# Attention output divided by broadcast sums on GpSimd instead of the probabilities, q turned in tile pairs, one unsplit unit, weights split in place

## The reference

```python
q_rot, k_rot = (rotate(q), rotate(k))
scores = scale * np.matmul(q_rot, k_rot.transpose(0, 1, 3, 2))
scores = scores - np.max(scores, axis=-1, keepdims=True)
attn = np.exp(scores)
attn = attn / (np.sum(attn, axis=-1, keepdims=True) + 1e-09)
return np.matmul(attn, v).astype(np.float32)
```

## Time and profile before

| | us |
|---|---|
| median of 3 runs | 1056.86 (1056.76 to 1062.91) |
| the profiled execution's own time | 1058.53 |
| its span, first to last instruction | 1056.7 |

### The profile page before, as it was taken

How to read it: one execution, slowest core, us unless ns; L and a number is a source line. 1 busy time by engine, 2 the same in 40 slices (tenths; PEclk the granted TensorE clock), 3 DMA queues, 4 the chain that set the end, 5 groups by cost and what they waited for, 6 DMA issues and landing times.

```text
span 1056.7 us, 21205 instructions
## 1 busy us (share of the span) xinstructions
PE 998.6 (94%) x7040; PEld 930.8 (88%) x7040; DVE 668.1 (63%) x1330; ACT 567.1 (54%) x1344; POOL 314.9 (30%) x317
## 2 busy tenths in 40 slices
PE   5888999998999998999999999999999999999997
PEld 4777777777888878999999999788999999999997
DVE  6999999999999997978666775455221221221220
ACT  4888999988999996444444442642131131121120
POOL 5777877877676721100000000342000000000000
PEclk9999999999999999999999999999999999999999
DMA  3122222222112101100000000130000000000000
GB/s 90 48 58 59 55 55 60 61 59 56 35 40 47 35 14 48 61 1 0 0 0 0 0 0 0 60 119 2 1 24 23 1 23 22 0 22 20 3 22 22
DMA packets 70078, 32.90 MB, mean 31 GB/s; under 512 B 62496, under 2 KB 63392, under 8 KB 70048
## 3 DMA queue, kind: packets, MB, share of 16 engines
q1 hardware_dynamic: 69760, 32.20, 11.4%
q10 hardware_dynamic: 288, 0.33, 0.1%
HBM read 27.79 MB, written 4.72 MB: 31 GB/s over the span
## 4 chain that ended last, share of the span: by engine, by line
PE 62%; DVE 18%; issue 11%; ACT 7%; DVEq 1%; DMA 0%; ACTq 0%; SPq 0%
PE psum L559 19%; PE psum L561 18%; PE psum L560 18%; DVE row_stats L974 4%; DVE pT_lo L991 3%; ACT probs L756 3%; DVE row_stats L997 2%; DVE probs L1004 2%; DVE pT_hi L991 2%; PE psum L530 1%; DVE qT L955 1%; ACT pT_hi L769 1%; PE psum L544 1%; DVE xT L1013 1%; PE psum L649 1%
## 5 line engine op out<-in xcount | busy, mean ns | idle before, releaser
L932 ACT ACTIVATE h_hi<-psum 128x288 fp32r<-128x288 f32 x96 | 39.5, 411 | 245.8 <-PE psum L561 245.8
L530 PE MATMUL psum<-ident,probs 128*128 128x128 f32 x800 | 138.4, 285 | 30.4 <-ACT pT_hi L769 12.9
L530 PEld LDWEIGHTS psum<-ident,probs 128*128 128x128 f32 x800 | 92.4, 142 | 55.7 <-ACT pT_hi L769 17.3
L974 DVE TENSOR_REDUCE row_stats<-psum 128x1 f32<-128x576 f32 (+1 forms) x160 | 119.9, 749 | 8.0 <-ACT probs L756 4.0
L1178 DVE SCALAR_TENSOR_TENSOR h_lo<-psum,h_hi 128x288 fp32r<-128x288 f32 x96 | 44.0, 458 | 125.8 <-ACT h_hi L932 125.8
L756 ACT ACTIVATE probs<-psum,row_stats 128x576 f32<-128x576 f32 (+1 forms) x160 | 118.8, 743 | 6.2 <-DVE row_stats L974 4.4
L559 PE MATMUL psum<-u_hi,wc_hi 128*128 128x288 f32 x384 | 114.3, 298 | 0.2 <-DVEq L1172 0.2
L559 PE MATMUL psum<-h_hi,wc_hi 128*128 128x288 f32 x384 | 113.7, 296 | 0.0
L560 PE MATMUL psum<-u_lo,wc_hi 128*128 128x288 f32 x384 | 113.3, 295 | 0.0
L560 PE MATMUL psum<-h_lo,wc_hi 128*128 128x288 f32 x384 | 113.3, 295 | 0.0
L561 PE MATMUL psum<-h_hi,wc_lo 128*128 128x288 f32 x384 | 112.9, 294 | 0.0
(11 more groups left out here) (137 smaller groups left out, 2940.1 us busy)
## 6 DMA issues: line engine op xcount, KB each, us to landing
stage_w<-in_moe_w_ch_dram SPq DMA_DIRECT2D x8, 768.0 KB, 4.4
out_dram<-stage_out SPq DMA_DIRECT2D x8, 576.0 KB, 3.7
raw_q<-in_q_dram SPq DMA_DIRECT2D x32, 128.0 KB, 2.2
raw_k<-in_k_dram SPq DMA_DIRECT2D x32, 128.0 KB, 2.3
raw_v<-in_v_dram SPq DMA_DIRECT2D x32, 128.0 KB, 2.1
stage_w<-in_moe_w_k_dram SPq DMA_DIRECT2D x4, 512.0 KB, 3.8
stage_w<-in_moe_w_v_dram SPq DMA_DIRECT2D x4, 512.0 KB, 3.5
raw_v<-in_v_dram SPq DMA_DIRECT2D x64, 16.0 KB, 2.0
```

The costliest lines, as they stand in the source:

```text
L530: ins = t.transpose(bank[:, at:at + P], probs[i][:, tile, at_key:at_key + P], ident[:, :])
L974: d_.tensor_reduce(neg_max[0:m, at:at + 1], score_banks[at][0:m, :, 0:HALF], AX.XY, ALU.max, negate=True).then_inc(maxed, 1)
```

## The change

- The probabilities are no longer divided. The inverse row sums (one `invert` per head, `I0`, all five tiles) go to a DRAM tensor `sum_rows` (`sums_out`, 640 single floats), come back broadcast over 64 partitions (`sums_back`, tile `rb`), and GpSimd multiplies the attention output of a pair of heads in place (`scale_x`, 576 wide, once per pair of slots). `N` steps are gone from both orders; `turn` waits for the exponentials alone.
- q is turned in pairs of tiles (three transposes, with k's tail tile as a fourth, `prepare` unit 0), then k's four full tiles (unit 1): two rounds where there were three (`PREP` 3). ScalarE and VectorE have four P steps each in place of three.
- Only unit 0 is whole; units 1, 4 and 5 are now split.
- q and k lie side by side in `raw_qk`, so GpSimd multiplies both by cos in one 640-wide instruction, and by sin in another.
- Gated weights load straight to where `w1_lo` lies (`w1_raw`) and are split in 20 pieces of 512, the last five after the loop of slots.
- The orders change: `v0` moves behind `E2` on ScalarE; `T1` moves ahead of `S0` on TensorE.

```diff
-    WHOLE = (1, 4, 5)
+    WHOLE = (0,)
-    ORDER = steps("T0 S0 T1 P0 S1 T2 V0 S2 T3 V1 V2 T4 P1 T5 S3 T6 V3 T7 V4 P2 V5 S4 V6 V7")
-    ACT_ORDER = steps("H0 H1 E0 N4 H2 P0 v0 H3 E1 O0 H4 P1 H5 E2 H6 H7 N1 P2 E3 O1 E4")
-    DVE_ORDER = steps("M0 L0 I1 N2 N3 M1 L2 P0 L3 M2 O0 I0 P1 N0 M3 L6 L7 P2 M4 O1")
+    ORDER = steps("T0 T1 S0 P0 S1 T2 V0 T3 V1 S2 T4 V2 T5 S3 P1 T6 V3 T7 S4 V5 V4 V6 V7")
+    ACT_ORDER = steps("H0 H1 P0 P1 P2 H2 E0 H3 E1 H4 O0 H5 E2 v0 H6 H7 P3 E3 O1 E4")
+    DVE_ORDER = steps("I0 M0 L0 L1 M1 P0 L2 P1 L3 M2 P2 L4 O0 L5 M3 L6 L7 M4 P3 O1")
-    LAST_DVE_ORDER = steps("I1 L0 N2 N3 X0 L2 X1 L3 O0 X2 X3 X4 L6 X5 L7 X6 O1 X7")
+    LAST_DVE_ORDER = steps("I0 L0 L1 X0 L2 X1 L3 O0 X2 L4 X3 L5 X4 L6 X5 L7 X6 O1 X7")
 ...
+            def sums_out(it, kk):
+                sp.wait_ge(sum_inv, upto(it, kk, 1, 1))
+                sp.dma_start(sum_rows[bass.ds(it * 2 + kk, 1), :].rearrange("o (t p) -> p (o t)", p=P),
+                             rsums[:, kk % 2, :], allow_slow_non_contiguous=True).then_inc(sums_stored, 16)
+            def sums_back(it, kk, first=False):
+                i = kk % 2
+                sp.wait_ge(sums_stored, it * 32 + (16 * kk + 16))
+                if i == 0 and not first:
+                    sp.wait_ge(x_scaled, it)
+                sp.dma_start(rb[i * D:i * D + D, :], sum_rows[bass.ds(it * 2 + kk, 1), 0:S].to_broadcast([D, S])).then_inc(rb_in, 16)
+            def slots(it, w=None, first=0, tiles=1, more=True, start=False):
+                if not start:
+                    sums_out(it, -1)
+                    next_v(it, 0)
+                    sums_back(it, -1)
+                if w is not None:
+                    load_w1(w, it, first, tiles)
+                if more:
+                    next_qk(it, 0)
+                sums_out(it, 0)
+                next_v(it, 1)
+                sums_back(it, 0, first=start)
+                if more:
+                    next_qk(it, 1)
 ...
+                g.tensor_tensor(times_cos[:, :, :, :], raw_qk[i][:, :, :, :], both(cos), ALU.mult).then_inc(rope_step, 1)
+                g.tensor_tensor(times_sin[:, :, :, :], raw_qk[i][:, :, :, :], both(sin), ALU.mult).then_inc(rope_step, 1)
+                pool.wait_ge(rope_step, upto(it, kk - 1, 2, 2))
+                for j, (rot, done) in enumerate(((rot_q[i], q_roped), (rot_k[i], k_roped))):
+                    g.tensor_tensor(*rope_half(rot, times_cos, times_sin, j, 0), ALU.subtract)
+                    g.tensor_tensor(*rope_half(rot, times_cos, times_sin, j, 1), ALU.add).then_inc(done, 1)
 ...
+            def scale_x(p):
+                pool.wait_ge(span_out, p * 4 + 4)
+                pool.wait_ge(rb_in, p * 32 + 32)
+                at = bass.ds(p * COLS + 1, S)
+                g.tensor_tensor(xT[:, at], xT[:, at], rb[:, :], ALU.mult).then_inc(x_scaled, 1)
 ...
+            def slots(it, n, scaling):
+                split_v(it, 0, 0)
+                rotate(it, 0, 2, False)
+                split_w1_hi(it, n)
+                pool.wait_ge(w_hi, it + 1)
+                split_v(it, 1, 1)
+                split_w1_lo(it)
+                rotate(it, 1, 3, False)
+                if scaling:
+                    scale_x(it - 1)
 ...
+                if unit == 0:
+                    if first:
+                        pe.wait_ge(first_roped, 2)
+                    else:
+                        pe.wait_ge(q_roped, upto(it, kk, 1, 1))
+                        pe.wait_ge(k_roped, upto(it, kk, 1, 1))
+                        pe.wait_ge(prep_lo, upto(it, kk, 4, 0))
+                    for p in range(PAIRS):
+                        t.transpose(prep_bank[:, p * P:(p + 1) * P], rot_q[i][:, 2 * p:2 * p + 2, :].rearrange("p a d -> p (a d)"), ident[:, :])
+                    ins = t.transpose(prep_bank[:, PAIRS * P:PAIRS * P + P], rot_k[i][:, FULL, :, :].rearrange("p a d -> p (a d)"), ident[:, :])
```

More of the change, by code:

```diff
@@ L347, in load_v, with load_w1 @@
                     sp.dma_start(raw_v[i][at:at + TAIL, FULL, 0:D], v_d[bass.ds(head, 1), FULL * P:S, :].rearrange("o p d -> p (o d)")).then_inc(v_in[i], 16)
[L349 to L352 removed]
+            def load_w1(w, it, first, tiles):
                 src = w[bass.ds(it * (tiles * P) + (-first * tiles * P), tiles * P), :].rearrange("(t p) n -> p t n", p=P)
[L354 removed]
@@ L356, in load_pair @@
[L356 to L365 removed]
+                sp.dma_start(w1_raw[:, bass.ds(it * UNIT, UNIT)].rearrange("p (t n) -> p t n", t=tiles), src).then_inc(w1_in, 16)
@@ L373, in _ @@
             sp.wait_ge(first_roped, 2)
-            load_pair(0, w_k, 0, 1, again=False)
+            load_qk(2, 0)
+            sp.wait_ge(k_roped, 2)
+            load_qk(3, 1)
+            slots(0, w_k, 0, 1, start=True)
             with sp.Fori(1, KD) as it:
-                load_pair(it, w_k, 0, 1)
+                slots(it, w_k, 0, 1)
             with sp.Fori(KD, N_WKR) as it:
-                load_pair(it, w_r, KD, 2)
+                slots(it, w_r, KD, 2)
             with sp.Fori(N_WKR, N_WV) as it:
-                load_pair(it, w_v, N_WKR, 2)
-            with sp.Fori(N_WV, HEADS // 2 - 1) as it:
-                load_pair(it)
-            sp.wait_ge(v_used, HEADS - 2)
-            load_v(HEADS - 1, 1)
+                slots(it, w_v, N_WKR, 2)
+            with sp.Fori(N_WV, HEADS // 2 - 2) as it:
+                slots(it)
+            slots(HEADS // 2 - 2, more=False)
+            last = HEADS // 2 - 1
+            sums_out(last, -1)
+            next_v(last, 0)
+            sums_back(last, -1)
+            sums_out(last, 0)
+            sums_back(last, 0)
+            sums_out(last, 1)
+            sums_back(last, 1)
             sp.wait_ge(span_out, 2 * HEADS)
@@ L453, in _ @@
             rotate(0, 1, 1, True)
-            with pool.Fori(0, N_WV) as it:
-                for i, split_w1 in enumerate((split_w1_hi, split_w1_lo)):
-                    split_v(it, i, i)
-                    rotate(it, i, i + 2, False)
-                    split_w1(it)
-            with pool.Fori(N_WV, HEADS // 2 - 1) as it:
-                for i in range(2):
-                    split_v(it, i, i)
-                    rotate(it, i, i + 2, False)
-            for i in range(2):
-                split_v(HEADS // 2 - 1, i, i)
+            def slots(it, n, scaling):
[8 more added lines that the diff above has]
+                    scale_x(it - 1)
+            slots(0, 1, False)
+            with pool.Fori(1, N_WV) as it:
+                slots(it, it + 1, True)
+            with pool.Fori(N_WV, HEADS // 2 - 1) as it:
+                slots(it, N_WV, True)
+            last = HEADS // 2 - 1
+            split_v(last, 0, 0)
+            for n in range(last, HALF_UNITS):
+                split_w1_hi(n, N_WV)
+                pool.wait_ge(w_hi, n + 1)
+                split_w1_lo(n)
+                if n == last:
+                    split_v(last, 1, 1)
+                if n == last + 2:
+                    scale_x(last - 1)
+            scale_x(last)
             for n, (size, sources, hi, lo, _) in enumerate(TOK_UNITS):
```

285 lines of the change are left out of this document (138 added, 147 removed).

## The result

The changed kernel takes 1165.28 us (median of 4 runs, 1164.4 to 1166.16) against 1056.81 for the kernel before, measured beside it: a ratio of 1.101, 95% interval 1.0974 to 1.1047. That is 108 us slower. The profiled execution took 1165.27, its span 1163.1.

A forecast was written before the change was run, and what follows sets the result against it. VectorE was taken to pace the kernel before (slot 12.0 us), a loop through GpSimd the changed one. 15 pairs of 29.25 us plus the ends gave +74.6 on 1058.5, 1133.1; less 1.7, 1131 us, range 1092 to 1166.

The forecast's parts named there:

- rival 4: Half clock in every attention slot, with stalls behind it: B = 8.0, slot pair 30.65, total 1152 us; chance 20%.
- The loop: In attention, P0 waits for values_hi, split_v and the whole rope: slot at least A plus B, pair 29.25 us; 48%.
- A: Part of a slot from the end of v on ScalarE to k roped on GpSimd: 6.70 us, odd heads 7.95.
- B: Part of a slot from TensorE's P0 to the end of the next v on ScalarE: 7.3 us.
- the warm B: B without clock loss: 6.1 us if ScalarE never waits, taken as 6.4 with small stalls.
- about 7 in 10 slots pay: Share of attention slots assumed to lose some 1.3 us in B to TensorE's half clock, giving B = 7.3.
- Ends: Outside the thirty intervals: v(0) +2.7 us, v(30) to v(31) 9.3, then 3.1 to the last half-slot, there -1.5.
- Cost nothing: Loads behind sums_out on SP's queue stay covered: no cost, or 0 to 2 us a pair if that cover went.
- Rival 1: No loop in attention, VectorE relieved: slot 10.7 us, 40 us less, total 1017 us; chance 5%.

The follow-up runs named there:

- the filler: The changed kernel with 24 extra transposes of the identity on TensorE ahead of P0's wait for the rope: 1145.49 us, ratio 1.0845 to the kernel before.

## Why the prediction was right, and where it was off

It said 1131, range 1092 to 1166, slower at 92%; the time is 1165. The mechanism is the one named, and the experiments bear out each link; the time came out at the top of the range, near rival 4: 1 us inside it, and that much is luck.

*The loop (48%).* Right. TensorE's P0 waits 3.0 and 4.3 us, its largest wait by far, as "3.2 to 4.5"; GpSimd runs without a gap from v_pair to the last half of k. VectorE fell to 67% ("about 70%"). Odd intervals are 1.4 longer than even ones, for 1.2.

*A.* Right to 0.03 us: 222.55 to 230.51 is 7.96 (7.95), 238.58 to 245.25 is 6.67 (6.70). The 640-wide product takes 1.56 (1.58 by the slope of the rows). The sum went by rows and not by the 1.41 of the Trainium skill's "GPSIMD Engine Reference", section Elementwise, which this trace doesn't bear out.

*B.* The term that was mis-sized, and with it all that attention missed: 438.75 us were forecast for the thirty intervals, 462.96 came. B was taken at 7.3; from k roped to the end of the next v it is 7.76 (214.79 to 222.55), 8.07 (230.51 to 238.58), and 8.1 on average over the thirty: 30 x 0.8 = 24 us. Two steps failed, each by about half of that.

The first is the warm B, "I take 6.4". With the clock held (the filler) it is 6.8. ScalarE's three P steps take 1.16 us from k's tail to H2, where the list had 0.76, and a stall of 0.17 stands before H4. In the filler kernel:

```profile
213.34 0.22 ACT L818 ACTIVATE kT_hi<-psum 128x64 fp32r<-128x64 f32 x1 [3.10 <-PE psum L575]
...
214.50 0.38 ACT L852 ACTIVATE pT_hi<-psum 64x256 fp32r<-64x256 f32 x1
```

The second is "I assume that about 7 in 10 slots pay". All thirty pay: each has a stretch at 0.50 on its way from P0 to v. The 1.3 us taken for one was right (8.1 - 6.8). The share was drawn from stalls of up to 1.6 us with a mean clock of 0.98, though the idles forecast were of the length of the 2.50 us one in rows 8, which did cost.

How long the clock stays down sets what a slot pays. In 23 of the thirty the stretch lasts 3.4 us, in seven 6.8, as here:

```profile
197.22:204.03 6.81, 4.34 (x16) 3.89 (x17) 2.16 (x4) 2.30 (x6) 3.73 (x5) 0.50 0.17 42
```

Those seven are the first interval and the odd ones of 16.4 to 16.9 us. Laid side by side over the changed kernel, the one with w_lo moved and the filler, the way from P0's start to the end of v is 6.7 us with no half clock in it (twice 7.1), 7.6 to 8.0 with 2.7 to 3.4 us of it, 8.3 to 8.5 with 4.2 to 4.6, 8.7 to 8.8 with 5.0 to 5.3, and 9.0 to 9.2 with 5.6 to 6.1. So the even intervals that rose to 15.9 are accounted for: a microsecond at half clock costs some 0.4 us.

*Rival 4 (20%)* had the better numbers, a B of 8.0 and a pair of 30.65, where the usual pair is 30.6 and the mean 30.86. So the 48% mechanism was right, and half clock in every slot came on top of it. Rival 4's 1152 lies 13 below: 3 for the longer intervals, the rest by the parts that follow.

*Ends.* v(0) 21.23 for 20.4; v(30) to v(31) 9.56 for 9.3; v(31) to the half-slot 3.54 for 3.1: 1.5 us together. From the half-slot to the end the time grew by 4.6 (1056.7 - 395.53 = 661.2; 1163.1 - 497.29 = 665.8) where -1.5 was forecast. In the first 10 us there TensorE is busy 4.2 us, before 6.6. The prediction counted the divisions that go, put GpSimd's last weight pieces at nothing, and left out the two more rests that VectorE must write. The rows show VectorE slowed while GpSimd works at those pieces (to 504.81); first before, then after:

```profile
397.82 0.95 DVE L1023 SCALAR_TENSOR_TENSOR mixed<-xT,mu,prev_part 128x288 f32<-128x288 f32 x2
398.85 0.46 DVE L1032 TENSOR_TENSOR xk_lo<-mixed,xk_hi 128x288 fp32r<-128x288 f32 x1
...
498.99 2.26 DVE L1098 SCALAR_TENSOR_TENSOR mixed<-xT,mu,prev_part 128x288 f32<-128x288 f32 x2
501.17 1.51 DVE L1107 TENSOR_TENSOR xk_lo<-mixed,xk_hi 128x288 fp32r<-128x288 f32 x1
```

With one more `xk_lo` of 1.52 that is 3.4 us, and TensorE waits 2.79 and 2.34 us for VectorE behind it. That this makes the 6.1 is read and not tested.

The misses add up: 24.2 + 1.5 + 6.1 = 31.8 us of the span. The rest of the 34 is the distance of the profiled execution to the median, 1.7 taken off and not there this time, and 0.4 between span and time.

*SP: "Cost nothing".* Right for this kernel (SP's order alone, 128 pieces alone), for a reason that doesn't hold elsewhere. The landing of `sums_out` was priced at 2.3 us from a load; it is 9 to 11. While v is late, the cover of the v loads is wide, that of the weights 0.6 to 1.9 us in eight pairs; with v first, the store decides: 1115 instead of 1014.

*Rival 1 (5%).* It didn't happen, but its time without a loop, a slot of 10.7 and 1017, is nearly met: with v first and 128 pieces the slot is 10.4 to 10.6 and the time 1014. So a gain of some 43 us lay behind two serial chains. How much of it the removed divisions hold isn't shown, and the match is in part luck. Over the last nine of the thirty intervals, where the kernel before has no weight pieces, the slot falls by 0.8 us (11.27 to 10.45); over the first twenty-one by 1.6 (12.30 to 10.71), where the pieces on GpSimd also became half as wide. (Its "14.3 here" for A + B fits neither 14.0 nor 14.6, what the prediction's own terms give for an even slot and on average.)

## What to carry to other kernels

Before an instruction is moved back in an engine's list, follow what stands *behind its consumer* in the consumer's queue, and ask whether that leads back to the instruction in the next round: such a loop sets the pace while no engine is full, and one more operand in a wait (here k) helps to close it. Removing one bound shows the next only; size the second from its own rows before promising what lies behind the first. A small store is priced by its number of separate pieces, and a kernel in which idles pull the clock down can hand back in one slot what an edit saved in another.

## What the runs showed of the hardware

- 640 separate 4-byte writes to DRAM take 9 to 11 us to land, 128 pieces of 16 or 20 B 1.8 to 1.9, a load of 512 separate floats 2.3. With the 640 in ScalarE's queue, 512 KB loads from SP's take 9.2 to 9.6 us in place of 3.7 to 3.8.
- Behind idles of 3.0 to 4.3 us in TensorE's work the granted clock was at 1.2 GHz for 3.4 us in 23 of 30 slots of the changed kernel and for 6.8 us in seven; with w_lo moved, for 6.8 us in every second slot, with the same idle of 2.99 us ahead. What decides between the two lengths stays open.
- fp32 transposes of the identity in the idle kept the clock up (0.986 and 0.994 of full speed over the run, against 0.943). In the filler kernel it fell five times before the last slot, each time in a slot that waited for weights.
- VectorE's addition of 1e-9 takes 0.17 us undisturbed. In the changed kernel it took up to 0.54 and twice 1.2 to 1.4, with v first and 128 pieces of 20 B up to 1.24, before up to 1.87. The Trainium skill, "SBUF — State Buffer", section Who interferes with whom, has the port pair of VectorE and GpSimd as an exclusive lock held for a whole instruction; this trace agrees: a 0.45 us one ends at 212.12, GpSimd's 640-wide product at 212.09.
